# The fullest expert of two batches goes first, with its weights loaded early and its first slot run beside the last routing

## The reference, cut to what matters

```
x = attention(q, k, v, M_prev, z_prev, beta)    # B=4, H=8, S=576, D=64 -> x is [2304, 512]
logits = x @ w_gate                             # 8 experts
e_idx = argmax(logits, axis=1)                  # one expert for each token
for e in range(8):                              # w1[e]: 512 x 1024, w2[e]: 1024 x 512
    h = relu(x[e_idx == e] @ w1[e]); out[e_idx == e] = gate * (h @ w2[e])
h = out @ w_in; out = (h - tanh(h)) @ w_out     # 512 x 2048, 2048 x 512
```

## Time and profile before

| what | us |
|---|---|
| median of three runs | 1030.22 |
| the profiled execution | 1030.83 |
| its span in the profile | 1029.0 |
| PE busy in the span | 996.1 (97%) |
| DVE busy | 645.9 (63%) |
| ACT busy | 503.6 (49%) |
| POOL busy | 474.0 (46%) |

### The profile page before, as it was taken

How to read it: one execution, slowest core, us unless ns; L and a number is a source line. 1 busy time by engine, 2 the same in 40 slices (tenths; PEclk the granted TensorE clock), 3 DMA queues, 4 the chain that set the end, 5 groups by cost and what they waited for, 6 DMA issues and landing times.

```text
span 1029.0 us, 16805 instructions
## 1 busy us (share of the span) xinstructions
PE 996.1 (97%) x5482; PEld 817.5 (79%) x5483; DVE 645.9 (63%) x1241; ACT 503.6 (49%) x1045; POOL 474.0 (46%) x334
## 2 busy tenths in 40 slices
PE   7999989899889999999999999999999999999998
PEld 4667758576547888888888879999999999999997
DVE  3777776877634444444444448777777777777664
ACT  6877777686235120022112047555555555655654
POOL 6665586775489833057537137332232322322221
PEclk9999999999889999999999999999999999999999
DMA  9555665431477443146482211010010010100001
GB/s 210 137 162 151 178 198 165 130 103 39 145 280 284 141 138 123 46 167 220 143 302 106 71 41 32 1 32 32 1 62 1 19 44 1 37 26 1 32 1 31
DMA packets 51009, 103.66 MB, mean 101 GB/s; under 512 B 7424, under 2 KB 16640, under 8 KB 50432
## 3 DMA queue, kind: packets, MB, share of 16 engines
q1 hardware_dynamic: 34416, 56.68, 19.0%
q10 hardware_dynamic: 13616, 36.70, 9.8%
q0 software_dynamic: 2912, 9.44, 3.0%
HBM read 82.62 MB, written 20.19 MB: 100 GB/s over the span
## 4 chain that ended last, share of the span: by engine, by line
PE 77%; DVE 6%; POOL 2%; issue 1%; ACTq 1%; ACT 0%; DVEq 0%
PE scores L1440 6%; PE scores L1442 6%; PE scores L1441 6%; PE scores L1381 5%; PE scores L1383 5%; PE scores L1382 5%; PE average L1396 4%; PE average L1395 4%; PE average L1394 4%; PE average L1272 2%; PE average L1457 2%; PE mix L1458 2%; PE turned L1457 2%; PE average L1458 2%; PE turned L1458 2%; PE mix L1457 2%
## 5 line engine op out<-in xcount | busy, mean ns | idle before, releaser
L574 POOL TENSOR_TENSOR g_lo<-g,g_hi 128x384 fp32r<-128x384 f32 x96 | 97.9, 1019 | 274.9 <-ACT g_hi L778 274.3
L537 POOL TENSOR_TENSOR ring<-ring 128x2048 fp32r<-128x2048 f32 x30 | 137.4, 4613 | 106.2 <-ACT ring L717 102.3
L717 ACT ACTIVATE ring<-ring 128x2048 fp32r<-128x2048 f32 x30 | 55.7, 1907 | 180.1 <-PE scores L1383 81.7
L1440 PE MATMUL scores<-yt_hi,w_in_hi 128*128 128x384 f32 x384 | 130.9, 341 | 1.7 <-DVE yt_lo L1131 1.7
L1442 PE MATMUL scores<-yt_hi,w_in_lo 128*128 128x384 f32 x384 | 129.2, 337 | 0.0
L1441 PE MATMUL scores<-yt_lo,w_in_hi 128*128 128x384 f32 x384 | 128.8, 335 | 0.0
L768 ACT ACTIVATE sq<-scores 128x384 f32<-128x384 f32 x96 | 47.2, 491 | 163.8 <-PE scores L1442 163.8
L1123 DVE COPY_PREDICATED ser<-big,th 128x384 f32<-128x384 int32 x96 | 118.9, 1239 | 3.3
L1118 DVE TENSOR_TENSOR ser<-ser,sq 128x384 f32<-128x384 f32 x96 | 55.9, 582 | 95.8 <-ACT ser L771 92.0
L600 ACT ACTIVATE prob<-scores,nmx 128x128 f32<-128x128 f32 (+3 forms) x128 | 66.4, 525 | 43.8 <-DVE nmx L853 40.8
L1381 PE MATMUL scores<-ring,xt_hi 128*128 x200 | 81.1, 406 | 3.1 <-POOL ring L537 1.7
(11 more groups left out here) (255 smaller groups left out, 2505.4 us busy)
## 6 DMA issues: line engine op xcount, KB each, us to landing
ring<-in_w ACTq DMA_DIRECT2D x13, 2048.0 KB, 9.0
q_sb<-in_qt SPq DMA_DIRECT2D x48, 288.0 KB, 4.2
k_sb<-in_kt SPq DMA_DIRECT2D x32, 288.0 KB, 4.3
xin<-x_sorted SPq DMA_DIRECT2D x27, 256.0 KB, 2.8
y_sorted<-y_sb SPq DMA_DIRECT2D x25, 256.0 KB, 2.1
v_sb<-in_v SPq DMA_DIRECT2D x16, 256.0 KB, 2.8
ring<-in_w SPq DMA_DIRECT2D x8, 512.0 KB, 4.1
w_out_sb<-in_w_out ACTq DMA_DIRECT2D x1, 4096.0 KB, 16.2
```

What stands on the lines that cost most here:

```text
L537: pool.tensor_tensor(ring[:, ring_at(k), 1, part], ring[:, ring_at(k), 1, part].bitcast(F32), ring[:, ring_at(k), 0, part].bitcast(F32), A ...
L574: pool.tensor_tensor(g_lo[:, t % GRING, :], g32[:, t % 2, :], g_hi[:, t % GRING, :].bitcast(F32), ALU.subtract).then_inc(g_lo_ok, 1)
L1440: mm(ff_h(t), w_h, yt_hi[:, j % 2, c, :], start=c == 0, stop=False)
```

## The change

The kernel takes the expert with the most rows in batches 0 and 1 as the first of the order and puts expert 0 in its place; every other expert keeps its place. With the counts above the order becomes 5, 1, 2, 3, 4, 0, 6, 7. Every weight address is now read from a register (`expert_of`). Further:

- `count` of batch 1 also counts the batch's total; DVE adds `largest` (four operations, n = 11, i = 4) and `order` (seven operations, n = 12, i = 1).
- The eight loads of 512 KB go out in n = 11 and n = 12, four in each; SP waits for `r_order` first.
- Units 0 and 1 are converted during n = 14, 15 and 16 in sixteen eighths (ACT), the last four low parts after `r_slots` (POOL).
- The rows of slot 0 are loaded when the last scores are done; they are transposed between the logits of the last batch and split by DVE before its pick.
- After the last count PE runs `first_up` in place of the 60 products, then `turn_hid(0)`, 9 products on ones and `first_down`, with the transposes of slot 1's rows in its middle.
- DVE signals `r_slots` when the rows' part of the table is done, then does relu(0) and split_hid(0), and only then the rest of the table.
- The table is built in the new order (`swap`, four operations, twice) and slots 2 to 6 are written out, so that the loop of six slots runs three times instead of four.
- POOL's scatters of batch 2's tiles 2 to 4 go after the loop.

```diff
+HIGH = {(14, 0): (0,), (14, 1): (1,), (14, 2): (2,), (14, 3): (3,), (15, 0): (4, 5), (15, 1): (6, 7), (15, 2): (8,), (15, 3): (9,),
+        (15, 4): (10,), (16, 0): (11, 12), (16, 1): (13, 14), (16, 2): (15,)}
+LOW_AHEAD = {14: (0,), 15: (3, 4, 5, 6, 7, 8), 16: (9, 10, 11)}
+LOW_BEHIND = {14: (1, 2)}
...
-                if 3 <= n < 3 + 2 * CD:
-                    load_first_expert(n - 3)
-
+                if n in (11, 12):
+                    if n == 11:
+                        sp.wait_ge(r_order, 1)
+                    first = sp.value_load(order_i[0:1, 0:1], min_val=0, max_val=E - 1)
+                    for c in range(CD):
+                        load_first_expert((n - 11) * CD + c, first)
+
+            row = sp.value_load(first_i[0:1, 0:1], min_val=0, max_val=E * REG)
+            sp.wait_ge(q_split, NP)
+            sp.wait_ge(scored, NP * QT)
+            sp.dma_start(xin[:, 0, :], xs[bass.ds(row, P), :]).then_inc(xin_ok[0], 16)
...
-                    if i == 3 and EARLY <= n < EARLY + 8:
-                        early_high(n - EARLY)
+                    for q in HIGH.get((n, i), ()):
+                        early_high(q)
...
-            for k in range(1, 3):
-                convert(k)
+            convert(2)
             act.wait_ge(scattered, 16 * TILES)
-            act.wait_ge(xin_ok[0], 16)
+            act.wait_ge(xin_ok[1], 16)
...
+            def largest():
+
+                rs(dve.tensor_reduce(first_s[:, 0:1], n_first[:, :], AX.X, ALU.max))
+                rs(dve.tensor_scalar(n_first[:, :], n_first[:, :], first_s[:, 0:1], None, ALU.is_equal))
+                rs(dve.tensor_tensor(n_first[:, :], n_first[:, :], desc[:, :], ALU.mult))
+                rs(dve.tensor_reduce(first_s[:, 1:2], n_first[:, :], AX.X, ALU.max))
+
+            def order():
+
+                rs(dve.tensor_scalar(chosen[:, :], desc[:, :], first_s[:, 1:2], None, ALU.is_equal))
+                rs(dve.tensor_tensor(order_f[:, :], chosen[:, :], expert_f[:, :], ALU.mult))
+                rs(dve.tensor_tensor(order_f[:, :], expert_f[:, :], order_f[:, :], ALU.subtract))
+                rs(dve.tensor_scalar(order_f[:, 0:1], first_s[:, 1:2], -1.0, float(E), ALU.mult, ALU.add))
+                dve.tensor_scalar(first_i[:, :], order_f[:, 0:1], float(REG), None, ALU.mult)
+                dve.tensor_scalar(base_o[:, :], order_f[:, :], float(REG), None, ALU.mult)
+                dve.tensor_copy(order_i[:, :], order_f[:, :]).then_inc(r_order, 1)
...
+            def swap(to, values):
+
+                rs(dve.tensor_tensor(part_e, values, chosen[:, :], ALU.mult))
+                rs(dve.tensor_tensor(to, values, part_e, ALU.subtract))
+                rs(dve.scalar_tensor_tensor(to, chosen[:, :], values[:, 0:1], to, ALU.mult, ALU.add))
+                rs(dve.tensor_reduce(to[:, 0:1], part_e, AX.X, ALU.add))
+
...
-            rs(dve.tensor_tensor(table[:, 2, :], row0, spare, ALU.subtract))
+            dve.tensor_tensor(table[:, 2, :], row0, spare, ALU.subtract).then_inc(r_slots, 1)
+            relu(0)
+            split_hid(0)
...
             for i in range(QT):
                 if i + 2 < QT:
                     turn_x((B - 1) * QT + i + 2, last_banks[i + 2])
                 pe.wait_ge(xl_act, (B - 1) * QT + i + 1)
                 logit(i, i % 4, t_ps[1], i * 2 * E).then_inc(logit_ok, 1)
+                if i == 2:
+                    turn_in(0, 0, o_ps[1])
...
+            first_up(up_at)
+            turn_hid(0)
+            idle_products(s_ps[0][0], AT_LAST)
+            first_down(down_at)
+            pe.wait_ge(r_table, 1)
+            up(1)
+            turn_in(0, 2, t_ps[0])
+            turn_hid(1)
+            for t in range(2, PEELED):
+                slot(t, t, (t + 1) // XIN)
```

More of the change, by code:

```diff
@@ L405, in store_y @@
                 sp.dma_start(ys[bass.ds(t * P, P), :], y_sb[:, k % 2, :]).then_inc(y_out[k % 2], 16)
-            for k in range(XIN):
+            for k in range(1, XIN):
                 load_x(k, k)
@@ L973, in _ @@
                     if 0 <= b < B - 1 and i == 2 and half == 3:
-                        place_rows(b, m_ps, RANKS)
+                        place_rows(b, m_ps, LOGITS if b == CHOICE else RANKS)
+                    if b == CHOICE and half == 3 and i == 4:
+                        largest()
+                    if b == CHOICE + 1 and half == 0 and i == 1:
+                        order()
                     if i == 0 and n >= 2:
@@ L1024, in _ @@
[L1024 to L1029, removed]
@@ new lines, in _ @@
+            dve.tensor_tensor(started[:, :, :], start_e[:, None, :].to_broadcast(wide),
+                              slot_f[:, :, None].to_broadcast(wide), ALU.is_le)
+            rs(dve.scalar_tensor_tensor(gap_o, start_e, -float(P), base_o[:, :], ALU.mult, ALU.add))
+            dve.tensor_copy(step_e[:, 0:1], gap_o[:, 0:1])
+            rs(dve.tensor_tensor(step_e[:, 1:E], gap_o[:, 1:E], gap_o[:, 0:E - 1], ALU.subtract))
+            begun, row0, unused, spare, from3, from4, from6, from8 = (small_t[:, r, :] for r in range(8))
@@ L1090, in _ @@
+            dve.tensor_tensor(table[:, 2, :], row0, spare, ALU.subtract).then_inc(r_slots, 1)
             relu(0)
-            split_x(1)
             split_hid(0)
-            with dve.Fori(0, (SLOTS - 1) // SPAN) as i:
-                for k in range(1, SPAN + 1):
-                    t = i * SPAN + k
-                    relu(t)
-                    split_x(t + 1)
-                    copy_y(i * SPAN + (k - 1), i * (SPAN // 2) + (k - 1) // 2, k - 1)
-                    split_hid(t)
+            rs(dve.tensor_reduce(unused2[:, :], unused[:, 0:SLOTS + 1].rearrange("p (k two) -> p two k", two=2), AX.X, ALU.add))
@@ new lines, in _ @@
+            split_x(1, t_ps[0])
+            dve.wait_ge(r_exp, 4)
+            gates_of(B - 1, B)
+            wide = [P, TILES, E]
+            swap(n_e, gap_o)
+            rs(dve.tensor_tensor(hot2[:, :, :], hot[:, 1:TILES + 1, :], n_e[:, None, :].to_broadcast(wide), ALU.mult))
+            rs(dve.tensor_reduce(row_f[:, 1, :], hot2[:, :, :], AX.X, ALU.add))
+            rs(dve.tensor_tensor(y_u[:, :], row_f[:, 0, :], row_f[:, 1, :], ALU.subtract))
+            for b in range(0, B, 2):
+                a, z = b * QT + QT - 1, (b + 1) * QT + QT - 1
+                dve.tensor_copy(y_u[D:P, a:a + 1], y_u[0:D, z:z + 1])
+                last = dve.tensor_copy(gate[D:P, a:a + 1], gate[0:D, z:z + 1])
@@ new lines, in _, with slot @@
+            rs(last)
+            dve.sem_inc(r_tails, 1)
+            def slot(t, at, half):
+                relu(t)
+                split_x(t + 1, t_ps[0])
+                copy_y(t - 1, half, at - 1)
+                split_hid(t)
+            copy_y(0, 0, 0)
+            relu(1)
+            split_x(2, t_ps[0])
+            split_hid(1)
+            for t in range(2, PEELED):
+                slot(t, t, (t - 1) // 2)
+            with dve.Fori(0, (SLOTS - PEELED) // SPAN) as i:
+                for at in range(PEELED, PEELED + SPAN):
+                    slot(i * SPAN + at, at, i * (SPAN // 2) + (at - 1) // 2)
```

234 lines of the change are left out of this document (136 added, 98 removed).

## The result

The changed kernel takes 1035.99 us (median of 18 runs, 1032.51 to 1039.93), against 1031.0 us for the kernel before in the same comparison (18 runs). The ratio is 1.0048, 95% interval 1.0039 to 1.0056. The forecast was 1032.3 us, its range 1024.5 to 1037: the time lies inside, near the upper end. The profiled execution's span is 1034.2 us, 5.2 us more than before.

A forecast was written before the change was run, and what follows sets the result against it. PE, busy 97% of the span, bounds the kernel, so only its waits or useless work can yield gains. Start -11.5, order +10.0 and attention +3.6 sum to +2.1 us: 1032.3 us, range 1024.5 to 1037.

The forecast's parts named there:

- The ring: Expert weight pipeline: PE waits 7.9 us for unit 14 before up(18), then 2.1 at low clock; loss 10.0 us.
- The start: First slot: its products replace the products on ones after the attention, up(2) at 310.7 against 322.2; gain 11.5 us.
- a bound (1.5): First slot: full clock in first_down's second half would add 1.5 us to the gain.
- The attention: Attention from n = 11 on: added operations and conversions lose 3.6 us, between 0.9 and 7.6.
- Part 3: The attention's delay: 0.85 + 1.3 + 0.7 + 0.8 = 3.6 us lost, between 0.9 and 7.6.
- the 7 us: Attention's end: prediction wrong if it moves by less than 1 or more than 7 us.
- the wait for q: Pair 13: q behind the order's wait and 2 MB of weights lands 216.5 to 224, needed near 217.
- rival (c): Pair 13: q lands late behind the weights, some 4 us more than the sum, 1036.5 us; chance 0.17.
- the likeliest case: Whole kernel: the forecast's own sum, +2.1 us, giving 1032.3; chance 0.47.
- `largest` and `order`: DVE at n = 11 and 12: four operations 0.85 us late; seven, the first held by POOL, charged 1.3.
- Pair 14: Attention, n = 14: three more eighths on ACT cost 0.7 us (0 to 1.5).
- Pair 15: Attention, n = 15: row cast and carry cast held by POOL's six eighths, 0.8 us (0 to 2.6).

The follow-up runs named there:

- Experiment 1: Changed kernel with the fullest expert first and those ahead of it moved back by one, instead of the swap; 1025.5 us, ratio 0.9951 to the kernel before.
- Experiment 2: Changed kernel with SP loading q of pairs 13 and 14 before the wait for the order and the weight loads; 1032.3 us, ratio 1.0016.
- experiments 4: Changed kernel with GpSimd's low eighths 1 and 2 moved from the end of pair 14 into pair 15's row of eight; 1039.13 us, ratio 1.0084.
- 5: Changed kernel with GpSimd's nine subtractions of pairs 14 and 15 left out, so its products are not right; 1034.29 us, ratio 1.003.
- experiment 8: Changed kernel with q loaded ahead of the weights, experts moved back by one instead of swapped, and GpSimd's subtractions spread; 1021.33 us, ratio 0.9895.
- 7: Changed kernel with q of pairs 13 and 14 loaded ahead of the weights and experts moved back by one instead of swapped; 1023.46 us, ratio 0.9919.
- experiment 6: Changed kernel with TensorE held before the first slot's products until slot 1's rows have landed; 1050.95 us, ratio 1.0179.

## Why the prediction was right or wrong

**The ring: right, in mechanism and size.** Forecast a wait of 7.9 and 2.1 for the clock; measured 8.0 and 2.0. The load came 11.8 us after up(16), where 11.7 was said. Experiment 1 takes all of it away.

**The start: right in mechanism, 3.5 us too small.** Forecast -11.5, measured -15.0. From first_up to up(2) the forecast had 31.0 us, the trace 27.7. Slot 1's rows came 0.9 sooner (16.6 instead of 17.5 us after first_up), and first_down's first half ended 1.0 later, so the wait was 1.69 us and not 3.5. The largest part, 2.0, is the clock: I took over the low clock that had followed the wait before, but after this shorter wait the granted clock stayed at 1.00. The forecast named this as a bound (1.5) and chose the other end. The last 0.4 is between up(1) and up(2).

**The attention: wrong, and the step that failed is Part 3.** Forecast +3.6, measured +10.0, beyond the 7 us at which the prediction called itself wrong. Its sum left the wait for q out and charged the held operations of pairs 14 and 15 too little.
- The wait for q was not in the sum. It was rival (c), at "some 4 us", and cost 3.96; the landing was forecast for 216.5 to 224 and came at 219.7. Its place, cause and price were right, and it should have been the likeliest case: the rows had q needed at 217, and the loads out until 211.4 with 9.2 us to land, which is 220.6. Experiment 2 takes the wait away and the time with it. The Trainium skill, "DMA: Bandwidth & Descriptors", section "Queues, rings and completion order", was cited for it (each DMA engine takes the descriptors of one ring in order), and q did stay behind the weights.
- `largest` and `order` were to cost 0.85 and 1.3; up to the mark of n = 13, 1.6 us are lost besides the wait, less than the 2.15 of the two together. The held operation was there, 2.57 us long, though not the first of the seven, which started at 204.73, ahead of GpSimd's subtraction.
- Pair 14: 0.7 forecast, 2.4 measured. I had counted ACT's conversions, which experiments 4 and 5 leave at most 0.5, and missed that GpSimd's subtractions 1 and 2 run beside the pick. These holds cost 1.9 at the high clock.
- Pair 15: 0.8 forecast, 1.9 measured. Both casts were held as said, for 1.7 us together, which fits the term's upper part.

The Trainium skill's rule that I weighed and left out of the sum ("SBUF — State Buffer", section "Who interferes with whom": VectorE operations with two inputs in SBUF are held by a GpSimd operation that reads SBUF) is borne out here: L965 and L989 are such ones and took 1.27 and 2.57 us. By it the pick's holds were to be foreseen.

The total came close by luck: the start's surplus (-3.5) covered half of the attention's (+6.4). In place of the likeliest case's +2.1 it is +5.2 in the span, and the median of 1035.99 is half a microsecond off rival (c)'s 1036.5 (4 us on 1032.3 make 1036.3). That is luck too: (c) has the start 3.5 us too slow and pairs 14 and 15 too fast.

## What to carry to other kernels

A load that moves behind a wait on a queue takes every later load of that queue with it: give each of them its landing time and the time at which it is needed, and where the two touch, that case is the likeliest. When work of one engine is moved, look at what the other engine that shares memory with it does at that very time, for all its small operations and not only the added ones. And where an order of buffers is changed, walk the ring with it: one swap of experts cost 10 us and a rotation, which makes the same choice, none. Two traces are compared from a mark that both share: the count of experiment 8 came 1.1 us earlier than that of 7, and the 1.1 us stood in the trace before the edit did anything.

## What the runs showed of the hardware

- A held VectorE operation lasts until GpSimd's ends, whatever its own size: eight elements took 2.57 us beside one of 2.67, and five elements 4.75 us, until the end of a row of eight subtractions (it began in the fifth). Another five elements beside a row of six took only 1.09, until the end of the fifth. What decides between the two isn't shown.
- Not every small operation beside a subtraction is held: in experiment 2 two of them (205.20 and 205.38) ran at 0.15 us while GpSimd's, begun at 205.14, was under way. They work on one element of each partition; the third, on eight, was held to its end. Whether the size decides was not tried. A reduction between the two held operations of the pick (L966 of the changed kernel, at 249.91) took 0.19 us while the second subtraction ran.
- TensorE's clock stayed at 2.4 GHz after a wait of 1.69 us, and was at 1.2 GHz after waits of 2.44 and, in experiment 6, 2.57 us. The length of the wait doesn't decide alone: first_up stood behind a wait of only 1.53 us, and its first ten products were 0.43 us apart; before that wait stood the small products of the logits. In experiment 8 the clock stayed up behind a wait of 1.75 us. The windows (the granted clock is the third number from the end): behind the wait in the changed kernel, then behind that of experiment 6.

```profile
306.20:309.40 3.20, 3.20 (x17) 2.69 (x18) 2.41 (x7) 0.00 (x0) 0.00 (x0) 1.00 0.75 189
```

```profile
306.40:310.00 3.60, 3.54 (x9) 2.83 (x10) 0.00 (x0) 0.00 (x0) 0.00 (x0) 0.54 0.78 226
```

- A load of q (288 KB) landed 8.5 us after its issue behind 2 MB of weights; the median of all loads of q in that profile is 3.9 us.
